# Gate and value products of the last stage issued term by term into two banks

## The reference

```
rms  = sqrt(mean(x * x) + 1e-6)
xn   = x / rms * rms_g                     # 3072 x 320
g    = xn @ w_gate                         # 320 x 1536
silu = g * (1 / (1 + exp(-g)))
val  = xn @ w_val                          # 320 x 1536
out  = (silu * val) @ w_out                # 1536 x 320
```

## Time and profile before

| | |
|---|---|
| median of 3 runs | 959.26 us (958.72 to 967.22) |
| the profiled execution | 959.15 us |
| its span, first to last instruction | 957.4 us |
| PE busy over the span | 880.5 us (92%) |
| DVE, ACT, POOL busy | 594.6, 388.2, 122.4 us |
| last stage, from the first gate product to the end | 549.2 to 957.4 us |

### The profile page before, as it was taken

The page is one execution under the profiler, slowest core; times in us unless marked ns, Lnnn a source line. Parts: engine busy times, 40 slices in busy tenths (PEclk is TensorE's granted clock), DMA queues, the critical chain, the costliest instruction groups (busy, mean ns, idle before and its releaser), DMA issues.

```text
span 957.4 us, 18376 instructions
## 1 busy us (share of the span) xinstructions
PE 880.5 (92%) x6073; PEld 780.6 (82%) x6097; DVE 594.6 (62%) x1270; ACT 388.2 (41%) x676; POOL 122.4 (13%) x167
## 2 busy tenths in 40 slices
PE   2999998985599999999999499999999999999997
PEld 1677776864499999999999288888888888888886
DVE  7489978996478877878877234445435435444332
ACT  5333222220477677777676223322331331332212
POOL 7244443343000000000000110100100100100000
PEclk9899688895599999999999699999999999999999
DMA  6544233312999899999996110100100100100000
GB/s 206 139 134 122 94 106 97 95 35 90 279 250 279 243 281 264 276 262 270 297 284 199 36 29 1 30 26 1 56 0 0 55 0 0 55 0 0 28 1 28
DMA packets 78171, 111.24 MB, mean 116 GB/s; under 512 B 11840, under 2 KB 56128, under 8 KB 78128
## 3 DMA queue, kind: packets, MB, share of 16 engines
q1 hardware_dynamic: 74672, 101.51, 36.8%
q0 software_dynamic: 2304, 7.88, 2.4%
q10 hardware_dynamic: 1152, 1.31, 0.4%
HBM read 95.32 MB, written 15.35 MB: 116 GB/s over the span
## 4 chain that ended last, share of the span: by engine, by line
PE 82%; DVE 9%; issue 3%; DMA 2%; SPq 1%; ACT 1%; DVEq 0%; POOL 0%; ACTq 0%; POOLq 0%
PE bank L1334 42%; PE bank L1409 4%; PE bank L1411 4%; PE bank L1410 4%; PE bank L1358 4%; PE bank L1360 4%; PE bank L1359 4%; PE bank L1266 2%; PE bank L1271 2%; PE bank L1224 2%; PE bank L1279 1%; DMA w_raw<-w 1%; DVE prob_T L879 1%; DVE qa L871 1%; PE bank L1216 1%
## 5 line engine op out<-in xcount | busy, mean ns | idle before, releaser
L1169 DVE TENSOR_TENSOR gated_lo<-gated,gated_hi 128x512 fp32r<-128x512 f32 x72 | 49.9, 693 | 184.7 <-ACT gated_hi L784 184.7
L779 ACT ACTIVATE sigm_sb<-bank 128x512 f32<-128x512 f32 x72 | 43.1, 598 | 254.4 <-PE bank L1334 242.3
L1334 PE MATMUL bank<-nT_hi,w_gv_hi 128*128 128x512 f32 x432 | 124.4, 396 | 2.6 <-DVE nT_lo L1156 2.6
L1334 PE MATMUL bank<-nT_lo,w_gv_hi 128*128 128x512 f32 x432 | 123.7, 395 | 0.0
L1334 PEld LDWEIGHTS bank<-nT_lo,w_gv_hi 128*128 128x128 f32 x432 | 81.7, 189 | 18.8
L633 POOL DMA_INDIRECT c_rows<-y_by_slot,slot_idx x24 | 22.8, 950 | 568.3 <-issue 305.6
L1334 PEld LDWEIGHTS bank<-nT_hi,w_gv_hi 128*128 128x128 f32 x432 | 79.2, 189 | 16.9 <-DVE nT_lo L1156 2.8
L1334 PE MATMUL bank<-nT_hi,w_gv_lo 128*128 128x512 f32 x288 | 90.9, 397 | 0.0
L1409 PE MATMUL bank<-w_out_hi,gated_hi 128*128 128x320 f32 x288 | 89.7, 311 | 0.0
L1411 PE MATMUL bank<-w_out_hi,gated_lo 128*128 128x320 f32 x288 | 89.1, 309 | 0.0
L1410 PE MATMUL bank<-w_out_lo,gated_hi 128*128 128x320 f32 x288 | 89.1, 309 | 0.0
(11 more groups left out here) (218 smaller groups left out, 1717.0 us busy)
## 6 DMA issues: line engine op xcount, KB each, us to landing
w_raw<-w SPq DMA_DIRECT2D x40, 640.0 KB, 6.8
w_raw<-w SPq DMA_DIRECT2D x40, 512.0 KB, 4.6
w_raw<-w SPq DMA_DIRECT2D x80, 128.0 KB, 5.0
kv_tok<-tok SPq DMA_DIRECT2D x24, 324.0 KB, 4.0
qk_sb<-qk SPq DMA_DIRECT2D x48, 160.0 KB
y_by_slot<-y_tile SPq DMA_DIRECT2D x12, 321.0 KB, 6.9
out_gate<-o_tok SPq DMA_DIRECT2D x4, 960.0 KB, 8.6
x_tile<-x_by_expert SPq DMA_DIRECT2D x12, 320.0 KB, 3.0
```

The source lines that it names most:

```text
L779: nc.scalar.activation(sigm_sb[f % 2][:], bank[2 * (f % 2)][:], ACT.Sigmoid).then_inc(sig_ready, 1)
L1169: dve.tensor_tensor(gated_lo[f % 4][:], gated[f % 2][:], gated_hi[f % 4][:].bitcast(F32), ALU.subtract).then_inc(hv_lo, 1)
L1334: m = mm(dst, w, x, start=(n == 0), stop=(n == len(terms) - 1))
```

## The change

The 16 matmuls of a block are issued in another order. The terms alternate between gate bank and value bank, and the group with the low weight comes before the group with the low input. Both waits stand ahead of the first matmul. The two increments of `gv_made` stay at the last matmul of the gate and of the value, which are now the 15th and the 16th. Nothing else is touched: `mm` is `nc.tensor.matmul`, and `passes` is still used by the expert stage.

```diff
             def gate_value(t, f):
                 n = NF2 * t + f
-                for v in range(2):
-                    c = slice(v * F2 + f * P, v * F2 + (f + 1) * P)
-                    if f >= 2:
-                        pe.wait_ge(silu_ready if v == 0 else hv_ready, n - 1)
-                    passes(bank[2 * (f % 2) + v][:], lambda k: w_gv_hi[:, k, c], lambda k: w_gv_lo[:, k, c],
-                           lambda k: nT_hi[:, k], lambda k: nT_lo[:, k]).then_inc(gv_made, 1)
+                if f >= 2:
+                    pe.wait_ge(silu_ready, n - 1)
+                    pe.wait_ge(hv_ready, n - 1)
+                cols = [slice(v * F2 + f * P, v * F2 + (f + 1) * P) for v in range(2)]
+                for k in range(KB):
+                    for v in range(2):
+                        mm(bank[2 * (f % 2) + v][:], w_gv_hi[:, k, cols[v]], nT_hi[:, k], start=(k == 0), stop=False)
+                for k in range(2):
+                    for v in range(2):
+                        mm(bank[2 * (f % 2) + v][:], w_gv_lo[:, k, cols[v]], nT_hi[:, k], start=False, stop=False)
+                for k in range(KB):
+                    for v in range(2):
+                        m = mm(bank[2 * (f % 2) + v][:], w_gv_hi[:, k, cols[v]], nT_lo[:, k], start=False, stop=(k == KB - 1))
+                        if k == KB - 1:
+                            m.then_inc(gv_made, 1)
```

## The result

The changed kernel takes 969.02 us (median of 20 runs, 962.21 to 982.70) against 959.57 for the kernel before beside it (20 runs, 956.27 to 968.19): 9.45 us more, 0.98%. The ratio, 1.0082 with a 95% interval of 1.0050 to 1.0114, leaves out executions more than 1.5% above a kernel's fastest, here three of the changed kernel's (978.55 to 982.70 us), and is smaller for it: 7.9 us more (4.8 to 10.9). The forecast was 968.5 us, 9.3 more.

A forecast was written before the change was run, and what follows sets the result against it. TensorE bounds the kernel, busy 30.00 of 30.00 us in the last stage. Terms 6.52 + 1.52 + 1.1 + 0.2 = 9.3 us on the profiled 959.15 gave 968.45, stated as 968.5; 8-in-10 range 965.5 to 974.

The forecast's parts named there:

- Part 2 and 3: Gate bank complete 1.63 us later; PE holes at tile ends: 6.52 us in tiles 1-4, 1.52 tile 0, 1.1 last.
- The covered places: Middle of a tile, cover of 3.9 us (bank reuse) and 3.7 (projection); tile's start, 0.4; the delay is free there.
- the signs that the prediction named: Last stage: five transpose waits of 1.5 to 1.6 us, 1.1 on the last projection, sigmoid 3.7 after the pair's start.
- Two signs of being wrong: From its list: 16 matmuls not taking 3.73 us, PE's last-stage idle not near 9 us, holes in a tile's middle.
- Part 4, the merged wait: Value's wait stands before the whole pair, 1.87 us earlier; only block 9 is late, 0.04 us, 0.2 in four loop tiles.
- Part 1, the matmuls: Each gate/value pair has 14 more changes of bank; cost bounded at -2 to +4 ns each, taken as 0.
- Rival one, the clock: Holes plus transposes at tile ends halve the clock, 1.4 us per fall: two 971.3, all five 975.5; chance 0.24.
- Rival two: Staying in one bank costs 0.020 us per matmul; 1,008 changes give back 20.2 us, total 948.2; chance 0.04.
- More than 4 ns per change: Inside the pairs, each change of bank costs over 4 ns; total 973 and above; chance 0.05.
- Rival three: The 0.13 us from product to transposes is mostly PE's own: holes 1.5, whole 8.5, total 967.7; no separate chance.
- Rival four: On the chip the gate's signal still comes after its eighth matmul; nothing moves, 959.3 us; chance 0.02.

The follow-up runs named there:

- The value first: Kernel before without alternation, the value's eight matmuls ahead of the gate's eight, the sigmoid waiting for the second signal; 971.21 us, ratio 1.0112.
- the one late signal: Kernel before, old order and banks, but one increment of two at the 16th matmul instead of one each at the 8th and 16th; 974.34 us, ratio 1.0112.
- the two kernels with block 11 set apart: Changed kernel with block 11 in the old order (957.74 us, ratio 0.9944); kernel before with only block 11 alternating (967.88 us, 1.0081).
- the high half first: Changed kernel, but ScalarE takes the high half of block f-1 ahead of the sigmoid of block f; 960.72 us, ratio 1.0012.
- the merged wait: As a run: kernel before, gate eight then value eight, with both waits ahead of the pair and low weight's terms before low input's; 960.20 us, ratio 0.9995.
- block 11 in turn: Changed kernel, but block 11 of each tile keeps the old order, gate eight then value eight, and old waits; 957.74 us, ratio 0.9944.
- the longer hole: Changed kernel, but the transposes at a tile's end wait for the low half of block 11 instead of its product; 980.31 us, ratio 1.0234.

## Why the prediction was right

The time (968.5 against 969.02), the sign and the range hold, and the main step, the holes at the tiles' ends, is the forecast one. That the two times lie within 0.5 us of each other is luck: the totals of one kernel spread by more than ten, the three measures of the loss are 9.45 (medians), 8.8 (last stage of the two profiles) and 7.9 us (ratio), and two small terms were wrong with opposite signs. By its steps:

- Part 2 and 3, the signal at the 15th matmul and the tile's end: 4 x 1.63 forecast, 4 x 1.64 in the trace; tile 0 1.52 against 1.49 (the transposes start 1.43 late and take 0.06 longer, 1.29 to 1.23 us by the starts of the matmuls ahead of and behind them); the last tile 1.1 against 1.17. The value first and the one late signal show that the place of the gate's last matmul makes this, not the alternation; the two kernels with block 11 set apart show that it is block 11; the high half first shows that the order on ACT and DVE makes 1.12 us of the chain.
- The covered places were covered: but for block 9, no wait in the middle or at the start of a tile. Of the signs that the prediction named, PE's waits are 8.1 us of "near 9", four of the five on the transposes last 1.54 and tile 0's 1.26, and the one on the last projection is 0.7 instead of 1.1 (0.10 and the slower beginning behind a wait stand ahead of it). Two signs of being wrong did show, both small: the 16 matmuls take 3.68 us and not 3.73, and the tile's middle has the late pair at block 9.
- Part 4, the merged wait, was too small: 0.04 forecast for block 9, 0.14 for its start and about 0.1 for its first matmuls measured, 1.0 us in four tiles instead of 0.2. Before, 1.72 us lay between block 7's product (728.84) and pair 9 (730.56); now the product ends at 748.42 and PE is free at 748.43, 1.71 less. And a wait that ends just late costs PE more than the lateness.
- Part 1, the matmuls, was put at 0 with a gain of 2 ns for each change of bank as the lower bound. The pair takes 3.68 instead of 3.71, the mean of 3.69, 3.72 and 3.73: 0.033 over 14 changes is 2.4 ns, just beyond that bound. The bound was too narrow in any case, as it allowed for rounding alone: the same three matmuls take 0.70 us at 741.50 and 0.68 at 730.56, and the prediction read one pair, the longest of the three. What it gives back can be read off from tile 1's transposes to PE's last matmul: 7.04 us more in all, where the terms give 6.56 + 1.17 + 1.0 = 8.7; so the 60 pairs there gave back 1.7, 0.028 each. With tile 0's 1.49 and 0.3 more in that tile, where alternating pairs take 3.73 us too and the clock at the start isn't the same, it makes the 8.8 of the stage. The term at 0 and the small one for block 9 were both too small, with opposite signs, and nearly cancel.
- Rival one, the clock, did not happen. What was named against it, that 1.63 us of idleness are short, fits the runs: with 2.93 us instead of 1.54 the clock fell at four ends, at 1.6 us each where 1.4 was forecast.
- Rival two, that staying in a bank costs 20 ns, is refuted in its size: the gain is an eighth of it. More than 4 ns per change as a loss is refuted too. Rival three's 8.5 us in all lies nearer the stage's 8.8 than the forecast's 9.3; but its holes of 1.5 don't fit, as the trace of one end, 1.64, speaks for the full 1.63. Rival four is refuted by the sigmoid's start, 3.65 us after the pair's instead of 2.07.

What stays open is why an alternating pair takes 3.68 us and one in turn 3.69, 3.72 or 3.73 (3.73 with the merged wait). It isn't the signal in the middle, since one late signal leaves 3.69, 3.72 and 3.73. Nor does the order inside the pair fix it, be it by the changes of bank or by neighbours that share their moving operand: block 11 in turn, between alternating pairs, takes 3.69 us in every tile (739.55 to 743.24 in its profile), and alternating pairs take 3.73 throughout tile 0 of the changed kernel, where the five other kernels that alternate in those blocks take 3.68. So the 2.4 ns are what a pair gained here, not a price of a change of bank.

## What to carry to other kernels

Interleaving two sums delays the first one by nearly the whole length of the second: look where the engine next to read it has its thinnest cover, and count from there, not from the steady state. Here 3.7 us of cover hid it in the middle of a tile, block 7 was left with none (pair 9 starts 0.14 late), and block 11 had none to begin with. Then look at what stands between on the readers' own queues: moving one instruction (the high half ahead of the sigmoid) took 1.12 of the 1.64 us away without touching TensorE.

## What the hardware showed that I had not expected

- Behind the longer hole the clock fell 0.65 us after the transposes had begun (0.4 to 0.7 at the four ends), 3.6 us after the last projection matmul had ended, so running transposes didn't keep it up; the 12 transposes alone, 1.5 us without a hole, never brought it down. The Trainium skill, TensorE: Matmul & The Clock Gate, Part 4: PE-mode transpose, says that a transpose doesn't count as busy in the way a matmul does. This run agrees, at 0.84 and then 0.50 of granted clock while they ran, but doesn't test it alone, since 2.93 us of idleness stood ahead of them.
- A pair of the same 16 matmuls takes 3.68, 3.69, 3.72 or 3.73 us. In the kernels with alternation the value holds over a stretch and can change over behind a wait: behind block 9's wait the changed kernel goes from 3.68 to 3.73 until the tile's end in two of the four loop tiles, and stays at 3.68 in the others.
- The first matmuls behind a wait take about 0.1 us longer than the same ones without: 1.47 instead of 1.37 us for six of 512 columns, 0.55 instead of 0.44 for three of 320.
- The totals of each kernel here spread by about 10 to 20 us from run to run. The profiles point to the stages ahead: the last stage's first matmul starts anywhere from 549.1 to 563.9 us, while two kernels that differ only in the projection's order agree within 0.01 us from tile 1 on.
